# When the first expert's row list is made: a list of five slots behind the fifth limit, or a list of three inside the fourth and fifth and a list of two inside the first expert stage

## What is computed

```python
X = np.fft.fft(np.fft.fft(x, axis=1), axis=2).real          # 9984 tokens of 256
logits = X @ w_gate                                         # 8 experts, cap = 1248 tokens each
for idx in np.argsort(-logits.flatten()):                   # greedy, the best pair first
    tok, e = idx // 8, idx % 8
    if assigned[tok] < 0 and counts[e] < cap: assigned[tok] = e; counts[e] += 1
Y[assigned == e] = relu(X[assigned == e] @ w1[e]) @ w2[e]   # first layer, exactly 1248 tokens an expert
out = second layer on Y: argmax expert, softmax weight x sigmoid gate, again relu(.. @ w1) @ w2
```

## Time and profile before

| | us |
|---|---|
| median of 3 runs (1362.03, 1362.06, 1365.91) | 1362.06 |
| the profiled execution's own time | 1359.75 |
| its span, first to last instruction | 1358.0 |

### The profile page before, as it was taken

The page is one execution under the profiler, slowest core; times in us unless marked ns, Lnnn a source line. Parts: engine busy times, 40 slices in busy tenths (PEclk is TensorE's granted clock), DMA queues, the critical chain, the costliest instruction groups (busy, mean ns, idle before and its releaser), DMA issues.

```text
span 1358.0 us, 30727 instructions
## 1 busy us (share of the span) xinstructions
PE 1278.2 (94%) x10398; PEld 1176.8 (87%) x10399; DVE 764.1 (56%) x2012; ACT 324.8 (24%) x787; POOL 571.4 (42%) x548
## 2 busy tenths in 40 slices
PE   8999899669999999899999998999999999999996
PEld 5667888548979888889899997999999999999996
DVE  5945888877586678875544544443333443433332
ACT  0013010023222323333332331222222222222221
POOL 5900011225665666565647441612443242544411
PEclk9999555579999999999999998999999999999998
DMA  8707232013212222222222221221232121232110
GB/s 336 253 30 268 100 135 86 2 31 109 85 56 75 65 75 66 68 73 82 62 83 75 73 85 41 81 75 39 78 104 76 39 84 60 77 106 75 47 39 20
DMA packets 63129, 115.98 MB, mean 85 GB/s; under 512 B 7736, under 2 KB 45377, under 8 KB 62912
## 3 DMA queue, kind: packets, MB, share of 16 engines
q1 hardware_dynamic: 39264, 72.16, 15.3%
q0 software_dynamic: 11808, 31.03, 6.9%
q10 hardware_dynamic: 11968, 11.63, 3.0%
HBM read 81.64 MB, written 34.45 MB: 85 GB/s over the span
## 4 chain that ended last, share of the span: by engine, by line
PE 74%; DVE 11%; issue 2%; DMA 1%; ACT 1%; POOL 0%; ACTq 0%; DVEq 0%; POOLq 0%; SPq 0%
PE bank L1123 22%; PE bank L1125 22%; PE bank L1124 21%; PE bank L1004 3%; PE bank L987 3%; DVE hot_r L1784 2%; PE bank L1272 1%; PE bank L1135 1%; DVE hot_q L1785 1%; DVE hot_q L1783 1%; DVE hT_low L1954 1%; DVE arena L1663 1%; DVE xT_low L1947 0%; PE bank L1015 0%; DVE arena L1728 0%
## 5 line engine op out<-in xcount | busy, mean ns | idle before, releaser
L1123 PE MATMUL bank<-weights_high,hT_high 128*128 (+1 forms) x1328 | 388.6, 293 | 0.0
L1125 PE MATMUL bank<-weights_high,hT_low 128*128 (+1 forms) x1328 | 378.4, 285 | 0.0
L1124 PE MATMUL bank<-weights_low,hT_high 128*128 (+1 forms) x1328 | 377.2, 284 | 0.0
L1123 PE MATMUL bank<-xT_high,weights_high 128*128 128x256 f32 (+2 forms) x1072 | 334.8, 312 | 9.2 <-DVE hT_low L1954 3.7
L1125 PE MATMUL bank<-xT_high,weights_low 128*128 128x256 f32 (+2 forms) x1072 | 330.7, 308 | 0.0
L1124 PE MATMUL bank<-xT_low,weights_high 128*128 128x256 f32 (+2 forms) x1072 | 329.8, 308 | 0.0
L1124 PEld LDWEIGHTS bank<-weights_low,hT_high 128*128 128x128 f32 x1328 | 250.4, 189 | 0.0
L1123 PEld LDWEIGHTS bank<-weights_high,hT_high 128*128 128x128 f32 x1328 | 250.2, 188 | 0.1
L1125 PEld LDWEIGHTS bank<-weights_high,hT_low 128*128 128x128 f32 x1328 | 250.2, 188 | 0.0
L1123 PEld LDWEIGHTS bank<-xT_high,weights_high 128*128 128x128 f32 x1072 | 204.2, 190 | 24.2 <-DVE hT_low L1954 7.4
L1125 PEld LDWEIGHTS bank<-xT_high,weights_low 128*128 128x128 f32 x1072 | 203.3, 190 | 11.3
(11 more groups left out here) (264 smaller groups left out, 1460.2 us busy)
## 6 DMA issues: line engine op xcount, KB each, us to landing
arena<-middle ACTq DMA_DIRECT2D x44, 258.0 KB
spectrum<-arena SPq DMA_DIRECT2D x39, 256.0 KB, 2.2
arena<-in_w2a_t SPq DMA_DIRECT2D x8, 1024.0 KB, 4.8
raw<-in_w1a SPq DMA_DIRECT2D x8, 1024.0 KB
raw<-in_w2a SPq DMA_DIRECT2D x8, 1024.0 KB
raw<-in_w1b SPq DMA_DIRECT2D x8, 1024.0 KB
raw<-in_w2b SPq DMA_DIRECT2D x8, 1024.0 KB
arena<-in_x SPq DMA_DIRECT2D x4, 768.0 KB, 4.2
```

Source lines behind the costliest of these rows:

```text
L1123: pe.matmul(out_, a[0], b[0], start=start, stop=False)
L1124: pe.matmul(out_, a[0], b[1], start=False, stop=False)
L1125: return pe.matmul(out_, a[1], b[0], start=False, stop=stop)
```

## The change

The five slots of the first list are divided. LISTS becomes ((0, 3), (3, 5), (5, 8)).

- Slots 0 to 2 (30 wide) are final when phase 2 has closed. Their list's preparation goes behind the compares of rounds 2 and 3 of phase 3 and behind its `accept`; the 13 batches go behind the compares of phase 4's rounds (2, 3, 3 and 3) and behind its `accept` (2). PE does the matmuls behind that round's `gate_parts`, ACT the scaling between the copies of the gates.
- `rows` comes right behind phase 4's count. `shut`, `reopen` and `slots` now follow it.
- Slots 3 and 4 (20 wide) are made in tiles 0 to 23: `running` at n = 0, `positions` at 2 and 3, batches at 4, 5 (two), 6, 8, 10, 14, 15, 16, 18, 20, 21, 22, `rows` at 23, `tokens` at 25. POOL waits for this list before it takes the row numbers of slot 3.
- The third list (slots 5 to 7) is as it was, in tiles 28 to 42.
- POOL issues the first four gathers before the last `add_given`, the last two splits and the split of the gates, and the next four behind them. PE's first hidden part waits for four splits of the weights instead of eight; the first result waits for all eight.

```diff
-LISTS = ((0, SERIAL), (SERIAL, E))
+EARLY = 3
+LISTS = ((0, EARLY), (EARLY, SERIAL), (SERIAL, E))
...
+BASE_AT = {0: 1, PLACES_AT: 2}
+TOKENS_AT = {GT - 1: 0, 25: 1, PLACES_AT + 16: 2}
+EARLY_AT = {(4, 0): (0, 1), (4, 1): (2, 3, 4), (4, 2): (5, 6, 7), (4, 3): (8, 9, 10), (4, ROUNDS): (11, 12)}
+WIDTHS = {1: dict(zip((4, 5, 6, 8, 10, 14, 15, 16, 18, 20, 21, 22), (1, 2, 1, 1, 1, 1, 1, 1, 1, 1, 1, 1))),
+          2: dict(zip(range(PLACES_AT + 4, PLACES_AT + 14), (1, 1, 1, 2, 2, 2, 1, 1, 1, 1)))}
...
@@ POOL
+            for u in range(NST):
+                pool.wait_ge(s_stored[u], 16 * len(range(u, NB, NST)))
+            pool.wait_ge(s_wlast, 16)
+            pool.wait_ge(s_blanked, 16 * (E + 1))
+            pool.wait_ge(m1.row, 1)
+            gathers(range(GT))
             add_given(SERIAL - 1)
             for c in range(c, SPLITS):
                 split(0, 0, c)
             pool.wait_ge(s_gates, E)
             split_gates(0, 0, expert_of(0))
...
-            gathers()
+            gathers(range(GT, 2 * GT))
@@ PE
+            def early_list(ph, r):
+                if (ph, r) == (EARLY, 2):
+                    prefix(bank[6][:, 384:384 + E], 1, s_pre)
+                for b in EARLY_AT.get((ph, r), ()):
+                    scatter(list_at(0), b, b, RING, hot_q, list_width(0), b == 0, b == BATCHES - 1)
             for ph in range(SERIAL):
                 for r in range(ROUNDS):
                     above_count(ph, r)
                     move(ph, r)
                     gate_parts(ph, r)
+                    early_list(ph, r)
                 new_count(ph, ind8)
                 gate_parts(ph, ROUNDS)
+                early_list(ph, ROUNDS)
...
-                            pe.wait_ge(m.split, e * SPLITS + SPLITS)
+                            pe.wait_ge(m.split, e * SPLITS + DCH * F // PW)
...
                     if k == 0:
+                        pe.wait_ge(m.split, e * SPLITS + SPLITS)
@@ ACT
+            for e in range(E - 2):
+                gates_of(e)
+            early_lanes(4, 0)
+            gates_of(E - 2)
+            for r in range(1, ROUNDS):
+                early_lanes(4, r)
+            gates_of(E - 1)
+            early_lanes(4, ROUNDS)
@@ DVE
+            def early_list(ph, r):
+                if (ph, r) == (EARLY, 2):
+                    slot_base(link, 0)
+                    dve.wait_ge(s_given, EARLY + 1)
+                    running(link)
+                if (ph, r) == (EARLY, 3):
+                    dve.wait_ge(s_pre, 1)
+                    link(dve.tensor_tensor(quota[:], quota[:], bank[6][:, 384:384 + E], ALU.add))
+                    positions(link, 0)
+                if (ph, r) == (EARLY, ROUNDS):
+                    positions(link, 1)
+                for b in EARLY_AT.get((ph, r), ()):
+                    one_hots(link, b, b, RING, hot_q, list_width(0))
...
                     compare(ph, r)
...
+                    early_list(ph, r)
...
                     mark(ph, r)
                     step(link, ph, r)
                 accept(link, ph)
+                early_list(ph, ROUNDS)
                 counted_new(link, ph)
...
-            (slots, slot_base, running, positions and 13 one_hots of 50 tiles, in one piece)
-            shut(link, open_log)
-            reopen(link)
             dve.wait_ge(s_hot_used, BATCHES)
             rows(link, list_at(0), *LISTS[0])
             dve.sem_inc(m1.row, 1)
+            shut(link, open_log)
+            reopen(link)
+            slots(link)
@@ DVE, routing(n): inside the expert stages
+                if n in BASE_AT:
+                    if n != PLACES_AT:
+                        dve.wait_ge(s_given, SERIAL + 1)
                     running(link)
-                    slot_base(link, 1)
+                    slot_base(link, BASE_AT[n])
```

More of the change, by code:

```diff
@@ L97 @@
 PLACES_AT = STEP[FINAL_AT + 1]
[L98 to L101, removed]
+BASE_AT = {0: 1, PLACES_AT: 2}
[3 more added lines that the diff above has]
+          2: dict(zip(range(PLACES_AT + 4, PLACES_AT + 14), (1, 1, 1, 2, 2, 2, 1, 1, 1, 1)))}
+BATCHES_AT = {n: (g, range(sum(w for m, w in at.items() if m < n), sum(w for m, w in at.items() if m <= n)))
+              for g, at in WIDTHS.items() for n in at}
+assert all(sum(at.values()) == BATCHES for at in WIDTHS.values())
 PIECES = [2, 2, 1, 1, 1, 1] + [0] * (TPE - 6)
@@ L735, in scatter1, with gathers @@
                                                 bounds_check=E * REG - 1, oob_is_err=False).then_inc(m.sent[gi], 16)
-                def gathers():
-                    indices(0, 0)
-                    for t in range(2 * GT):
+                def gathers(tiles):
+                    if 0 in tiles:
+                        indices(0, 0)
+                    for t in tiles:
                         if t >= GT:
@@ L1058, in scatter @@
                 mm.then_inc(s_hot_used if ring == RING else s_slow_used, 1)
-            for b in range(BATCHES):
-                q = list_width(0)
-                scatter(bank[2][:, 0:2 * q].rearrange("p (o q) -> p o q", o=2), b, b, RING, hot_q, q, b == 0, b == BATCHES - 1)
+            def early_list(ph, r):
[3 more added lines that the diff above has]
+                    scatter(list_at(0), b, b, RING, hot_q, list_width(0), b == 0, b == BATCHES - 1)
+            for ph in range(SERIAL):
+                for r in range(ROUNDS):
+                    above_count(ph, r)
+                    move(ph, r)
+                    gate_parts(ph, r)
+                    early_list(ph, r)
+                new_count(ph, ind8)
+                gate_parts(ph, ROUNDS)
+                early_list(ph, ROUNDS)
             last_read = [None]
@@ L1346, in _, with gates_of @@
             act.sem_inc(m1.y, 2)
-            for e in range(E):
+            def gates_of(e):
                 act.wait_ge(s_gates_ps, e + 1)
@@ L1407, in expert @@
                             if fast:
-                                for b in BATCHES_AT.get(e * TPE + FIRSTS[gi] + j, ()):
-                                    lanes(BATCHES + b, RING, hot_q, list_width(1))
+                                g, now = BATCHES_AT.get(e * TPE + FIRSTS[gi] + j, (0, ()))
+                                for b in now:
+                                    lanes(g * BATCHES + b, RING, hot_q, list_width(g))
                             y_out(e, gi, j)
@@ L1838, in _ @@
                     shut(link, src)
-            slots(link)
-            slot_base(link, 0)
-            dve.wait_ge(s_given, SERIAL + 1)
-            running(link)
-            dve.wait_ge(s_pre, 1)
-            link(dve.tensor_tensor(quota[:], quota[:], bank[1][:, 0:E], ALU.add))
-            for part in range(2):
-                positions(link, part)
-            q = list_width(0)
-            for b in range(BATCHES):
-                one_hots(link, b, b, RING, hot_q, q)
+            dve.wait_ge(s_hot_used, BATCHES)
+            rows(link, list_at(0), *LISTS[0])
+            dve.sem_inc(m1.row, 1)
             shut(link, open_log)
             reopen(link)
-            dve.wait_ge(s_hot_used, BATCHES)
-            rows(link, bank[2][:, 0:2 * q].rearrange("p (o q) -> p o q", o=2), *LISTS[0])
-            dve.sem_inc(m1.row, 1)
+            slots(link)
             on_limit = Count(dve, s_limit)
```

74 lines of the change are left out of this document (31 added, 43 removed).

## The result

The changed kernel takes **1373.22 us** (median of 4 runs, 1372.09 to 1373.72) where the kernel before takes 1362.74 (4 runs beside it): ratio 1.0073, interval 1.0059 to 1.0088. The forecast was 1373.4, slower. The profiled execution of the changed kernel is 1373.72, its span 1371.9, so what lies outside the span is 1.8, as before.

What follows compares the result with a forecast made beforehand. DVE was taken to bound the stretch from phase 4's count to the first list's end, PE a calm expert stage. The terms -2.4 + 1.7 + 12 = +11.3 on the median 1362.06 gave 1373.4 us, range 1361 to 1384.

Steps and rivals of the forecast that it cites:

- The mark of phase 4's last round: Phase 4's round 3 mark comes 24.3 us later, near 275.8 instead of 251.46: preparation 4.05, eleven batches 14.5, POOL 5.7.
- the meeting with POOL: Phases 3 and 4: five new DVE pieces beside POOL's four splits and one add_given lose 5.7 us, between 0 and 6.85.
- From the mark to `rows`: End of phase 4: PE's queue, ACT's scalings and the last matmuls put `rows` 10.15 us behind the last mark.
- Behind `rows`: After the first list: `shut` delays POOL's row-number copy 0.7, add_given, splits and gates come 1.0 late; together +1.7 us.
- Preparation in tiles 0 to 3: Second list's preparation, 5.9 us of work where DVE is full, costs 5 us: 4.8 without POOL, up to 7 with it.
- The 13 batches: Second list's batches in the stages cost 7 us, DVE's share and PE's 4.4 of matmuls together.
- Stages 0 to 2 together: Sign of being right: these stages 10 to 14 us longer, from a forecast list cost of 12; under 6 would be wrong.
- Slot 3's stage: Where the list of slots 5 to 7 is made, 73.5 us before; slots 3 to 7 were to be unchanged.
- side 1: Phase 4's last mark to the first list's end: 34.45 against 36.85 us, a gain of 2.4.
- the first (DVE has room): Rival: POOL waits, the stages pay only PE's 4.4, under 4 us lost decides for it; 1357 to 1358, chance 0.10.
- the second: Rival: both sides give halves, 5 us gained at side 1, 6 lost in the stages; +1, 1363, chance 0.15.
- The fourth's ring wait: Rival: early list's batches wait for buffers behind PE's gate parts, 0.4 a round, 1.5 us; rival's chance under 0.02.

Runs made afterwards that it cites:

- a_no_list: Changed kernel without the list of slots 3 and 4: no batches, running count, prefix, base or positions for it; 1359.00 us, ratio 0.9977 to the kernel before.
- a_no_batches: Changed kernel without the 13 batches of the list of slots 3 and 4, its preparation kept; 1368.05 us, ratio 1.0048 to the kernel before.
- a_fill: Changed kernel with dummy matmuls in PE's two new waits, 20 ahead of tile 1's prefix and 18 ahead of hidden part 3; 1372.04 us, ratio 1.0082.
- a_best: Changed kernel with POOL's order of before, second list's preparation in tiles 4 to 7, first list's tokens ahead of the first x_out; 1374.24 us, ratio 1.0104.
- a_pool_before: Changed kernel with POOL's order of before: add_given, two splits and the gates' split ahead of all gathers; 1376.73 us, ratio 1.0116.
- b_gathers_first: Kernel before with POOL's order alone changed: first four gathers ahead of the last splits, PE waiting for four splits, not eight; 1360.24 us, ratio 0.9990.
- a_tokens_early: Changed kernel with the first list's tokens moved from tile 3 to DVE's queue ahead of the first x_out; 1375.09 us, ratio 1.0084.

## Why the prediction was right, and where its terms were off

- **The mark of phase 4's last round.** Forecast: 24.3 us later, near 275.8. Measured 277.68, less the 2.0 by which this trace is late from the start: 275.7. Of its three parts the meeting with POOL is 5.4 for 5.7, and the other two together 18.8 for 18.55. The Trainium skill, SBUF — State Buffer, § Who interferes with whom, has DVE and GpSimd exclude each other there, whoever issues first; the trace agrees at 262.68 to 264.96: first the split waits for `hot_r` (1.97 for 1.26), then DVE's next instruction for the split (1.29 for 0.35).
- **From the mark to `rows`.** Forecast 10.15 (its own terms add up to 10.3), measured 8.66. Three batches' matmuls took 1.06, not 3 x 0.64, a figure that no row shows, and the last ones and the scaling were somewhat shorter. So the gain was 3.95, not 2.4.
- **Behind `rows`.** Forecast +1.7 (0.7 for the copy of the row numbers and 1.0 for the rest), measured +0.8. The copy wasn't late at all: 0.95 behind `rows`, against 1.09 before. The rest was near its forecast of 1.0: phase 5's first three compares, beside POOL's `add_given` and splits, took 4.40 for 2.89, and not all of that reached tile 0.
- **Preparation in tiles 0 to 3.** This is the term that was mis-sized: 5 forecast, **9.0** measured (a_no_list against a_no_batches). The step that failed is "Added are the 5.9 of preparation; less the idle, and with nothing for POOL: 4.8", taken as 5 where its own upper end was 7. What it sized too small is POOL: the instructions of the preparation take 9.0 us of DVE's time in tiles 0 to 3, where the forecast has 5.9, for the scan, `tot_b` and the `positions` instructions are stretched beside POOL's splits (1.05 for an 8-element cast, 1.90 where 0.81 was the time alone). The first `h_out` comes 6.3 us later behind tile 0 than before, the shorter tokens taken off; and from that `h_out` to tile 4's result it is 15.5 where it was 12.9, in which the clock stood at 0.52 and 0.62 for 4 us. At those levels about 1.7 us of full-speed work is lost. That the clock costs this much here wasn't shown by removal, since a_fill didn't keep it up there; only its like in a_best was. The signs fit only in sum: PE's part 3 waited 2.41 for DVE, 1.8 more than before and not 5, but PE had already waited 2.69 at tile 1.
- **The 13 batches.** Forecast 7, measured 3.4 to 5.8, around the 4.4 that the forecast has for PE's matmuls alone: DVE's share was mostly hidden.
- **Stages 0 to 2 together** were to be 10 to 14 longer. From tile 0 to tile 30 they are 8.9 + 1.6 + 0.9 + 4.2 = 15.6 longer, outside that band by the preparation.
- **Slot 3's stage** was to be unchanged and is 1.8 shorter (71.7 for 73.5). This isn't the list: a_pool_before, with the same work there, has 73.6, b_gathers_first 73.4, a_no_list 71.3. The rows put all of it between the results of tiles 39 and 40, 18.25 us before and 16.38 now. There a batch of the third list stands beside POOL's next split of weights. In the kernel before two of its three instructions are held up more (1.39 and 1.36 us at 589.66 and 590.98, for 0.60 and 0.95 at 603.49 and 604.01), and PE waits 0.29 us for DVE's `place_i` and 1.20 for that batch's scaling; in the changed kernel it waits for neither. So it is again the meeting of DVE and POOL, decided by how the two fall against each other at that moment, and nobody forecast it.

So the sum, +11.3, met the measured 10.5 by luck in part: errors of both signs cancelled. By the traces: side 1 gave 1.55 more than forecast, behind `rows` 0.9 less was lost, slot 3's stage gave 1.8, and stages 0 to 2 took 3.6 more than the 12; 11.3 - 1.55 - 0.9 - 1.8 + 3.6 = 10.65. The mechanism and the sign were right (the list in the stages costs more than the serial part gives, shown by taking it away); a sum's closeness says little of its terms.

Of the rivals, the first (DVE has room) needed under 4 us of loss in the stages, and the second some 6, where 13 to 15.6 were measured. The fourth's ring wait was 0.46, once (at 280.31), and POOL waited 0.41 for slot 3's rows (at 476.24), with no splits or gathers held up for long.

## What to carry to other kernels

Work taken from a serial stretch into a stage bounded by another engine is priced by the next hand-over to that engine, not by the mean share of busy time: DVE was at 56%, yet 6 us of its work cost 9 in tiles 0 to 3, and 5 to 6 in tiles 4 to 7 (with the batches set closer). Look at the stretch between two things that the bounding engine waits for, and count the instructions in the queue there. A wait put into PE may cost little, where PE must wait again soon behind it (a_fill), or its length and then half speed as well, where nothing behind it takes it up (a_best).

## What the runs showed of the hardware that was not expected

- A DVE instruction with a single SBUF input (TENSOR_SCALAR, 128x30 f32) stood for 4.81 us in a_tokens_early, behind an indirect transfer's issue and three POOL instructions in a row, though it began ahead of all three (292.69; they at 293.21 and from 294.97). So POOL's back-to-back instructions passed a waiting DVE instruction here. The Trainium skill, SBUF — State Buffer, § Who interferes with whom, has it that a `tensor_scalar` can take the shared ports, and the trace fits that; its rule that the order of issue decides who waits doesn't fit this row.
- The granted clock fell from 1.00 to 0.5 behind waits of 2.4 to 2.7 us in a PE that was otherwise busy (319, 336), and stayed there for some 3 us; in a_best it fell behind two smaller waits (1.67 and 0.92) ahead of the first hidden part, where the 0.92 alone left it at 1.00 in a_pool_before. Once it cost 2.8 us, once nothing, because PE would have waited for DVE behind it anyway.
